# Cluster masks by column tiles and VectorE block transposes, attention unrolled, its last units interleaved with the rational products

## What is computed

```python
# attention: B=2, H=8, S=768, D=64, C=16 clusters
c_n = centroids / (norm(centroids) + 1e-6)               # q, k alike
q_assign = argmax(einsum('bhsd,hcd->bhsc', q_n, c_n)); k_assign = argmax(... k_n ...)
scores = where(q_assign == k_assign, q @ k.T / sqrt(D), -1e9)
x = softmax(scores) @ v                                  # -> x [1536, 512]
# rational layer
h = x @ w_in                                             # [1536, 2048]
P = a0 + a1 h + a2 h^2 + a3 h^3;  Q = 1 + |b0||h| + |b1| h^2
y = (P / (Q + 1e-6)) @ w_out                             # [1536, 512]
# bilinear layer
out = ((y @ w1) * (y @ w2)) @ w3 @ w4
```

## Time and profile before

| | before |
|---|---|
| median of 3 runs | 807.36 us |
| the profiled execution: its own time | 805.25 us |
| its span | 803.4 us |
| busy: TensorE, VectorE, ScalarE, GpSimd | 774.8, 448.6, 409.3, 325.4 us |
| chain that ended last: TensorE's share | 93% |
| one exponential (L1066), one row maximum (L1276) | 808, 963 ns |
| one cast of q or k (L1030), one `g_rest` (L539) | 796, 1298 ns |
| mean granted TensorE clock | 0.98 |

### The profile page before, as it was taken

The page is one execution under the profiler, slowest core; times in us unless marked ns, Lnnn a source line. Parts: engine busy times, 40 slices in busy tenths (PEclk is TensorE's granted clock), DMA queues, the critical chain, the costliest instruction groups (busy, mean ns, idle before and its releaser), DMA issues.

```text
span 803.4 us, 10853 instructions
## 1 busy us (share of the span) xinstructions
PE 774.8 (96%) x3761; PEld 605.7 (75%) x3761; DVE 448.6 (56%) x767; ACT 409.3 (51%) x662; POOL 325.4 (41%) x229
## 2 busy tenths in 40 slices
PE   5899999999999969999999999999999999999998
PEld 4677677677765637888888888887888888888886
DVE  6778888888875175676877687666432111110120
ACT  4366677677675475888767677774221011101101
POOL 0067677767767533765122123443341210210220
PEclk8699999999999989999999999999999999999999
DMA  8423423433331070200000002521100000001001
GB/s 203 114 68 89 103 70 89 104 83 90 94 76 30 21 229 2 73 1 0 1 1 1 0 1 105 209 105 39 68 0 1 1 26 27 1 14 39 0 0 52
DMA packets 51947, 44.80 MB, mean 56 GB/s; under 512 B 28576, under 2 KB 43200, under 8 KB 51904
## 3 DMA queue, kind: packets, MB, share of 16 engines
q1 hardware_dynamic: 49744, 41.29, 18.4%
q10 hardware_dynamic: 2160, 2.95, 1.3%
HBM read 28.35 MB, written 3.15 MB: 39 GB/s over the span
## 4 chain that ended last, share of the span: by engine, by line
PE 93%; DVE 2%; ACT 2%; DMA 1%; POOL 1%; issue 1%; SPq 0%; ACTq 0%; POOLq 0%
PE psum L812 89%; PE psum L817 3%; PE psum L600 1%; ACT P L1066 1%; DVE psum L1276 0%; DVE OPS L1188 0%; DMA RAWQK<-in_k 0%; POOL PSUMS L1390 0%; DMA XT<-XL 0%; PE psum L889 0%; DVE MROW L1276 0%; ACT OPS L1048 0%; ACT OPS L1047 0%; SPq L776 0%; ACT TT L393 0%
## 5 line engine op out<-in xcount | busy, mean ns | idle before, releaser
L812 PE MATMUL psum<-OPS 128*128 128x384 f32 x576 | 133.7, 362 | 8.0 <-DVE psum L1276 2.7
L1390 POOL TENSOR_TENSOR PSUMS<-PSUMS,P 128x768 f32<-128x768 f32 x64 | 117.2, 1832 | 39.2 <-ACT P L1066 39.0
L812 PE MATMUL psum<-XT,W 128*128 (+1 forms) x576 | 131.0, 389 | 0.0
L539 POOL TENSOR_TENSOR G<-TT,G 128x512 fp32r<-128x512 f32 x48 | 62.3, 1298 | 165.0 <-ACT G L417 165.0
L812 PEld LDWEIGHTS psum<-OPS 128*128 128x128 f32 x576 | 98.5, 194 | 40.1 <-issue 23.4
L812 PEld LDWEIGHTS psum<-XT,W 128*128 128x128 f32 x576 | 108.1, 188 | 22.4
L1066 ACT ACTIVATE P<-psum 128x768 f32<-128x768 f32 x96 | 77.6, 808 | 60.1 <-PE psum L812 59.0
L1276 DVE TENSOR_REDUCE psum<-psum 128x1 f32<-128x768 f32 x90 | 86.7, 963 | 35.3 <-PE psum L812 35.3
L714 DVE TENSOR_TENSOR ABF<-AS,psum 128x512 f32<-128x512 f32 x24 | 16.5, 687 | 146.8 <-ACT AS L688 146.8
L738 POOL TENSOR_TENSOR W<-ABF,W 128x512 fp32r<-128x512 f32 x24 | 30.9, 1288 | 147.2 <-DVE W L718 147.2
L812 PE MATMUL psum<-G,WSPLIT 128*128 128x512 f32 x360 | 86.6, 390 | 1.1 <-POOL G L539 1.1
(11 more groups left out here) (118 smaller groups left out, 1154.4 us busy)
## 6 DMA issues: line engine op xcount, KB each, us to landing
OPS<-OPS SPq DMA_DIRECT2D x32, 192.0 KB, 3.0
W3R<-in_moe_w SPq DMA_DIRECT2D x8, 512.0 KB, 3.4
W12RAW<-in_moe_w SPq DMA_DIRECT2D x8, 512.0 KB, 3.7
RAWQK<-in_q SPq DMA_DIRECT2D x16, 192.0 KB, 3.1
RAWQK<-in_k SPq DMA_DIRECT2D x16, 192.0 KB, 3.2
XT<-XH SPq DMA_DIRECT2D x32, 96.0 KB, 2.1
XT<-XL SPq DMA_DIRECT2D x32, 96.0 KB, 2.1
out<-OS SPq DMA_DIRECT2D x12, 256.0 KB, 2.0
```

Of the source, the lines that this page charges most:

```text
L539: nc.gpsimd.tensor_tensor(G[:, n % 2, 1, :], TT[:, n % 4, :], G[:, n % 2, 0, :].bitcast(F32), ALU.subtract).then_inc(g_lo, 1)
L812: return nc.tensor.matmul(o, stationary, moving, start=start, stop=stop, skip_group_check=True)
L1390: nc.gpsimd.tensor_tensor(total, P32[:, (2 * u[1]) % 4, :] if n == 1 else total, P32[:, (2 * u[1] + n) % 4, :], ALU.add).then_inc(p_added, 1)
```

## The change: what it does

- `similarities` now takes the centroids (32 columns, 16 of them zero) as the stationary operand and 384 rows of q or k as the moving one, in plain float32, four products into four column tiles of 32. The similarities come out transposed.
- VectorE turns them in 32x32 blocks (`turn_similarities`), and turns the one-hot matrix back the same way (`turn_one_hot`); `masks` on TensorE, `round_similarities` and `clusters_first` go. ScalarE scales (`scale_masks`): for units 0 and 1 straight into OPS in four instructions, for the others in one into `MROWS`, from which SP places it by four DMAs and a fifth that restores three rows (`place_masks`). The turned similarities and masks lie in the bank of SUMS, where the similarities lay before.
- `place_maxima` is one DMA in place of three. Loads of V move from ScalarE's queue to SP's.
- `v_over_tiles` moves from VectorE to GpSimd (three additions), `round_v_sums` from VectorE to ScalarE. GpSimd writes constants into OPS at the start (eight memsets).
- Attention is unrolled, unit order is by batch, and the orders inside the steps change. Units 14 and 15 are written out with `early_product` 0 to 3 and the elementwise work of blocks 0 to 2 between their parts; loads of weights 6 to 10 come earlier.

```diff
-                for n in range(2 * NT):
-                    last = mm(tiles[:, n], ops(u, AQ if n < NT else AK)[:, (n % NT) * P:(n % NT + 1) * P],
-                              CT[:, head_of(u)[1]].rearrange("p s c -> p (s c)"), True, True)
+                for g in range(4):
+                    last = mm(sims_bank(u)[g * QUAD:(g + 1) * QUAD], CT[:, h, :],
+                              ops(u, (AQ, AK)[g // 2])[:, g % 2 * HALF:(g % 2 + 1) * HALF].bitcast(F32), True, True)
...
+            def turn_similarities(u):
+                dve.wait_ge(sims_ready, u + 1)
+                if has(u - 4):
+                    dve.wait_ge(x_made, u - 3)
+                if has(u - 1):
+                    dve.wait_ge(masks_copied, u)
+                nc.vector.transpose(SIM, sims_bank(u)).then_inc(sims_read, 1)
...
+            def turn_one_hot(u):
+                dve.wait_ge(one_hot, u + 1)
+                nc.vector.transpose(SIM, MASK.rearrange("p t c -> p (t c)")).then_inc(masks_turned, 1)
...
+            def scale_masks(u):
+                act.wait_ge(masks_turned, u + 1)
+                if u < DIRECT:
+                    for part in range(4):
+                        last = nc.scalar.activation(ops2(u, (BQ, BK)[part // 2], slice(D, D + QUAD))[:, part % 2, :],
+                                                    SIM[part * QUAD:(part + 1) * QUAD, :], ACT.Copy, scale=BIG_ROOT)
+                else:
+                    if u > DIRECT:
+                        act.wait_ge(mask_rows, 80 * (u - DIRECT))
+                    last = nc.scalar.activation(MROWS, SIM, ACT.Copy, scale=BIG_ROOT)
+                last.then_inc(masks_copied, 1)
...
+            def place_masks(u):
+                sp.wait_ge(masks_copied, u + 1)
+                for side, which in ((0, BQ), (1, BK)):
+                    for x in range(2):
+                        part = (2 * side + x) * QUAD
+                        sp.dma_start(OPS[D:D + QUAD, u % 4, which, x * HALF:(x + 1) * HALF].bitcast(F32),
+                                     MROWS[part:part + QUAD, :].bitcast(F32)).then_inc(mask_rows, 16)
+                sp.dma_start(OPS[96:99, u % 4, BQ, :].bitcast(F32), OPS[99:102, u % 4, BQ, :].bitcast(F32)).then_inc(mask_rows, 16)
```

More of the change, by code:

```diff
@@ L806, in _ @@
+            place_x(UNITS - 2)
+            for f in range(10, 14):
+                load_later_weights(sp, f)
+            place_x(UNITS - 1)
+            load_later_weights(sp, 14)
+            load_later_weights(sp, 15)
             later_loads(sp)
@@ L953, in _ @@
[L953 to L968 removed]
+            sides(1)
@@ new lines, in _ @@
+            similarities(0)
+            sides(2)
+            similarities(1)
+            for n in range(NT):
+                score_max(0, n)
+            similarities(2)
+            sum_v(0)
+            turn_maxima(0)
+            score_max(1, 0)
+            score_max(1, 1)
+            scores(0, 0)
+            sides(3)
+            score_max(1, 2)
+            empty_values(0)
+            scores(0, 1)
+            score_max(1, 3)
+            scores(0, 2)
+            score_max(1, 4)
+            scores(0, 3)
@@ L1015, in _ @@
-            early_product(EARLY - 1)
-            probs_v((3, 3), 2)
-            sums((3, 3))
+                sum_v(u + 1)
+                score_max(u + 2, 2)
+            for u in range(1, UNITS - 2):
+                step(u)
+            scores(14, 0)
+            early_product(0)
+            scores(14, 1)
+            score_max(15, 3)
+            probs_v(13, 2)
+            scores(14, 2)
+            score_max(15, 4)
+            sums(13)
+            empty_values(14)
+            scores(14, 3)
@@ new lines, in _ @@
+            score_max(15, 5)
+            probs_v(14, 0)
+            scores(14, 4)
+            turn_maxima(15)
+            sum_v(15)
+            probs_v(14, 1)
+            scores(14, 5)
+            early_product(1)
+            scores(15, 0)
+            early_product(2)
+            scores(15, 1)
+            probs_v(14, 2)
+            scores(15, 2)
+            sums(14)
+            empty_values(15)
+            scores(15, 3)
+            probs_v(15, 0)
+            scores(15, 4)
+            early_product(3)
@@ L1018, in _ @@
+            scores(15, 5)
+            probs_v(15, 1)
+            probs_v(15, 2)
+            sums(15)
             rational_products(pe, mm, lambda n: transpose_w3(pe, n))
@@ new lines, in _ @@
+            absolute(act, 1)
+            round_x(13)
+            exponent(15, 1)
+            take_out(14)
+            exponent(15, 2)
+            hidden(act, 2)
+            exponent(15, 3)
+            logarithm(act, 1)
+            reciprocal_guess(act, 1)
+            exponent(15, 4)
+            reciprocal_sums(14)
+            round_g(act, 0)
+            exponent(15, 5)
+            hidden(act, 3)
+            absolute(act, 2)
+            take_out(15)
+            round_x(14)
+            reciprocal_sums(15)
@@ L1151, in _ @@
+            logarithm(act, 2)
+            round_g(act, 1)
+            reciprocal_guess(act, 2)
+            rational_scalar(act, round_x)
             bilinear_scalar(act)
```

972 lines of the change are left out of this document (506 added, 466 removed).

## The result

The changed kernel takes 778.17 us (776.9 to 778.41, four runs); the kernel before, on the same chip, 807.87. The ratio is 0.9626 [0.9609, 0.9644]: 29.7 us less, where 780.0 was forecast. The profiled execution took 778.41 us, its span 776.5, 26.9 less than before.

The account below looks back on a forecast made before the run. TensorE was taken as the bound, busy 774.8 of 803.4 us. Steady part 10.6, start 4 and end 12.5 sum to 27.1 us off the 807.36 median: 780.3, forecast 780, range 771 to 796.

Parts of the forecast that it names:

- The bound: Whole kernel: TensorE is busy 774.8 of 803.4 us, so only shortening its queue or its 28.6 us idle moves the time.
- The similarities: Steady units, main term: 1.83 us leave TensorE's queue, four side-by-side products add 0.80; unit from 15.58 to 14.55 us.
- The two rivals in which a call overlaps only the next, or none: Similarity products: overlapping only the next, 1.77 us, total 793.9, 8%; none side by side, 2.76 us, total 811, 3%.
- The new wait: Steady step: score_max(u+2, 0) waits for five mask DMAs on SP; rows there at 10.2 us, TensorE asks at 10.24.
- both waits: Steady steps: mask-row wait and scores-exponential wait, together given 0.2 us a unit, bounds 0 and 1.1.
- The wait between scores and exponential: Steady steps: the next scores wait 1.04 us for the exponential; the new order leaves 1.20, covered by 0.16.
- the rival with late mask rows: Steady steps: costs 13 steps times the delay; 790 at 3.0 us landing, 816 at 5; faster 13%, slower 3%.
- The start: Before step 1: first maxima some 2 us earlier, scores(1, 0) at 44.5 instead of 48.64; -4 us (0 to -6).
- the chain is row maximum, bank free, next maxima: Start, up to step 1: what sets the pace there, without the sum of V and two steps of similarities.
- The end: End of attention into the rational layer: 11.2 us idle plus 3.5 of low clock; -12.5 us (-14.7 to -4).
- The cover: End of attention: other work fills each wait, nothing stands over 0.5 us; rival: not covered, 788.5 us, 11%.
- The 2.2 us given back for steps mis-ordered: End of attention: allowance taken off the 14.7 us at most to be had, leaving 12.5.

Follow-up runs that it names:

- 3: The changed kernel with the four similarity products issued twice, tiles in turn (0 1 2 3 0 1 2 3): 786.11 us, ratio 0.9753.
- 6: The kernel before the change with the six mask transposes of each unit issued twice: 817.81 us, ratio 1.0134.
- experiment 4: The changed kernel with the four similarity products issued twice, ordered by tile (0 0 1 1 2 2 3 3): 787.0 us, ratio 0.9758.
- Experiment 2: The changed kernel with the mask DMAs issued later in SP's step, after copy_rows(u+3): 812.74 us, ratio 1.0068.
- 7: The changed kernel with unread identity products filling TensorE's gaps in the first 35 us: 777.51 us, ratio 0.9634.
- 9: The changed kernel with mask DMAs issued before place_x and ScalarE's wait for the rational layer's coefficients moved behind unit 0's sixth exponential: 774.09 us, ratio 0.9589.

## Why the prediction was right, and where its terms were off

- **The bound.** "Only what shortens its queue" held: slots taken off (the change), added to the new kernel (3: 0.66 us a unit by its rows) and added to the old one (6: 0.64) all moved the unit by their length.
- **The similarities.** Forecast 0.80 us and a unit of 14.55; 0.78 and 14.59. Four tiles side by side was inferred from two; experiment 4 agrees with it: the queue does not hold a free tile back. The two rivals in which a call overlaps only the next, or none, fall with it.
- **The new wait** was the mis-sized term of the steady part. The chain was seen with no slack; the 0.2 us a unit that both waits were given was too little: 178.86 - 12 x 14.59 = 3.8 us, 0.3 a unit, all of it the mask rows (the unit's 0.04 us over the forecast make another 0.5). It is not even: six units wait, the others don't. SP's timeline shows why; the columns are start, length, instruction:

```profile
155.43 2.51 SPq L759 DMA_DIRECT2D OPS<-MROWS  x4
...
170.02 3.30 SPq L759 DMA_DIRECT2D OPS<-MROWS  x4
173.36 0.72 SPq L761 DMA_DIRECT2D OPS<-OPS  x1
...
185.37 2.76 SPq L759 DMA_DIRECT2D OPS<-MROWS  x4
```

  Four issues of masks take 2.51 us in the unit before, which does not wait, 3.30 here, and 2.76 in the next, which waits a little (its period is 14.83). In five of the six units that wait, one of the four issues takes 1.2 to 1.6 us and the others some 0.6; in the sixth, the last one shown, there is a pause of 0.4 us between two issues. The fifth issue begins at 173.36, and TensorE goes on at 175.45, 2.09 later; the forecast had 2.1 to landing. In a unit without a wait that distance is 2.23, so the slack was some 0.15 us. The wait between scores and exponential, which shared the 0.2, cost nothing in these steps. Experiment 2 shows the forecast's other side: the rival with late mask rows was right in sign, and too cheap, because it took the delay alone, and not the clock behind it, nor that some of the waits grew longer than the delay.
- **The start** was 2.7 us, not 4. The first maxima came as forecast; "the chain is row maximum, bank free, next maxima" left out the exponential, which in step 0 has only a maximum of 0.41 us to cover a turn-around of 1.04 (two waits of 0.55). It also took the clock of before for granted and asked nothing of the price of a clock that stays low: the filling alone, in 7, brings the second unit's maxima forward by 1.75 us, more than the 1.4 by which `scores(1, 0)` came late. ScalarE's wait for the coefficients was overlooked too, but at the low clock it costs nothing (9).
- **The end** gave 16.1 us, 13.1 forecast. Step 13, up to `scores(14, 0)`, gave 0.7 of them (0.6 forecast, the masks), and what follows 15.4, more than the 14.7 that the forecast called the most to be had. The cover held at each place: 0.60 us of TensorE stands still in the stretch, of 11.2, so idle time gave 10.6. Busy time gave the other 5.5, by the windows: 3.5 is the clock's, as worked out from the earlier trace rows; 0.6 the masks of step 13; 1.4 is left, of which 0.4 are in the slots of the four early products (11.0 us together in place of 11.4) and the rest is not followed. The 2.2 us given back for steps mis-ordered were the mis-sized term: nothing was mis-ordered.
- The errors have different signs: 1.3 and 2.0 us too much, 3.0 too little. The sum, 26.9 in spans for 27.1, is nearer than its terms deserve: that is luck.

## What to carry over

When one engine is full, its slots are a price list: read the slot and not the record, and add. When a change adds a wait on a DMA, write down the chain in the issuing queue and put the transfer that has no slack first; here the place of one call in SP's order moved the time between 773.7 and 812.7 us. An in-order queue that waits for something wanted much later blocks what is wanted now, and where a removed limit shows no gain, look for a second one over it before giving it up.

## What the hardware showed that was not expected

- Column tiles of TensorE start out of the order of the program when their tile is free (experiment 4: one record of each of four tiles in flight at the begin, 13 ns apart in the records, though four records of the first tile stood ahead).
- A DMA issue on SP takes 0.6 us as a rule, and 1.2 to 1.6 us now and then (at 67.0, 82.2, 126.5, 171.3 and 214.8 us in the changed kernel, five of the masks' 56 issues from MROWS). What delays it stays open.
- A stop of TensorE of 2.27 us was followed by 6.8 us at 1.2 GHz; of stops of 1.56 to 1.57 us some were followed by 3.4 us of it and others by none, and one of 2.03 us by none (experiment 2). What decides stays open.
